# Building per-expert row lists block by block, in place of one sort at the end, in a fused attention, dense and expert kernel

## The reference

```python
# 1 local attention: 4 batches, 8 heads, 768 positions, 64 wide
for each chunk of 32 positions:
    keys = 8 memory keys + the chunk, 16 positions before it, 8 behind it
    a = softmax(q_chunk @ keys.T / 8);  out_chunk = a @ values
x = out as [3072, 512]
# 2 dense layer: w_in 512x2048, w_out 2048x512
h = x @ w_in;  x = (h * cos(h)) @ w_out
# 3 routed experts: 8 experts, w1[e] 512x1024, w2[e] 1024x512
rows = x @ w_skip > 0                   # the other rows stay as they are
e = argmax(x @ w_gate);  gate = softmax(x @ w_gate)[e]
out[rows] = x[rows] + gate * (relu(x[rows] @ w1[e]) @ w2[e])
```

## Time and profile before

| what | value |
|---|---|
| median of 3 runs | 877.75 us (876.94 to 879.12) |
| the profiled execution | 877.95 us, its span 876.3 us |
| mean granted TensorE clock | 0.973 |
| PE busy | 819.5 us, 94% of the span |
| DVE, ACT, POOL busy | 520.9, 469.0, 50.2 us |
| chain that ended last | PE 87%, DVE 5%, ACT 2%, DMA 2%, issue 2% |
| SP's loads of raw expert weights | 512 KB each, 5.6 us to landing |

### The profile page before, as it was taken

One profiled execution on the slowest core, in us unless ns is written; L12 is line 12 of the kernel. 1 busy time (PEld: TensorE's weight loads), 2 busy tenths in 40 slices (PEclk: granted clock), 3 DMA queues, 4 the chain that ended last, 5 costly groups with the idle time before them and its releaser, 6 DMA issues.

```text
span 876.3 us, 20405 instructions
## 1 busy us (share of the span) xinstructions
PE 819.5 (94%) x8018; PEld 725.3 (83%) x8019; DVE 520.9 (59%) x1030; ACT 469.0 (54%) x809; POOL 50.2 (6%) x57
## 2 busy tenths in 40 slices
PE   5799999999999999999999999999982989999995
PEld 3688888898888888888888888898961878999994
DVE  3677655655565655556555655654458577666664
ACT  3577665565566555555655565563461555444442
POOL 0000000000000000000000000000014022111110
PEclk9799999999999999999999999999995899999998
DMA  9822031104213210422132031020053375655653
GB/s 337 298 82 68 25 109 62 61 25 134 65 58 106 65 61 27 119 76 61 60 111 61 26 108 62 25 73 1 1 195 89 128 279 193 215 201 224 231 205 118
DMA packets 40690, 97.42 MB, mean 111 GB/s; under 512 B 5852, under 2 KB 5852, under 8 KB 40608
## 3 DMA queue, kind: packets, MB, share of 16 engines
q1 hardware_dynamic: 37632, 90.21, 30.3%
q0 software_dynamic: 2976, 6.05, 1.9%
HBM read 82.34 MB, written 16.79 MB: 113 GB/s over the span
## 4 chain that ended last, share of the span: by engine, by line
PE 87%; DVE 5%; ACT 2%; DMA 2%; issue 2%; POOL 0%; SPq 0%; POOLq 0%; DVEq 0%; ACTq 0%
PE h_ps L721 30%; PE y_ps L735 29%; PE h_ps L822 9%; PE y_ps L837 7%; PE s_ps L625 2%; PE s_ps L662 2%; PE turn L686 1%; PE turn L676 1%; DMA xg<-x_mid,idx_from 1%; PE turn L640 1%; DMA k_pre<-qk 1%; PE turn L696 1%; DVE w_lo L1262 1%; PE turn L807 1%; PE s_ps L807 0%
## 5 line engine op out<-in xcount | busy, mean ns | idle before, releaser
L721 PE MATMUL h_ps<-xT_hi,in_hi 128*128 128x384 f32 x512 | 181.5, 354 | 1.7 <-DVE xT_lo L1067 1.4
L721 PE MATMUL h_ps<-xT_hi,in_lo 128*128 128x384 f32 x512 | 173.5, 339 | 0.0
L721 PE MATMUL h_ps<-xT_lo,in_hi 128*128 128x384 f32 x512 | 173.0, 338 | 0.0
L735 PE MATMUL y_ps<-out_hi,g_hi 128*128 128x512 f32 x384 | 150.0, 391 | 5.0 <-DVE g_lo L1144 5.0
L735 PE MATMUL y_ps<-out_hi,g_lo 128*128 128x512 f32 x384 | 152.1, 396 | 0.0
L735 PE MATMUL y_ps<-out_lo,g_hi 128*128 128x512 f32 x384 | 151.6, 395 | 0.0
L901 ACT ACTIVATE hs<-h_ps 128x384 f32<-128x384 f32 x128 | 62.5, 488 | 156.1 <-PE h_ps L721 155.9
L1138 DVE TENSOR_SCALAR whole<-us 128x384 f32<-128x384 f32 x128 | 45.3, 354 | 131.8 <-ACT us L902 131.8
L925 ACT ACTIVATE us<-us 128x384 f32<-128x384 f32 x128 | 67.2, 525 | 73.2 <-DVE us L1140 72.9
L721 PEld LDWEIGHTS h_ps<-xT_hi,in_hi 128*128 128x128 f32 x512 | 97.2, 190 | 5.3 <-DVE xT_lo L1067 1.8
L721 PEld LDWEIGHTS h_ps<-xT_lo,in_hi 128*128 128x128 f32 x512 | 97.4, 190 | 1.6
(11 more groups left out here) (156 smaller groups left out, 1209.3 us busy)
## 6 DMA issues: line engine op xcount, KB each, us to landing
raw<-w SPq DMA_DIRECT2D x72, 512.0 KB, 5.6
k_sb<-qk SPq DMA_DIRECT2D x22, 512.0 KB, 4.5
v_sb<-v SPq DMA_DIRECT2D x22, 512.0 KB, 3.5
x_mid<-x SPq DMA_DIRECT2D x24, 256.0 KB, 5.2
out<-x SPq DMA_DIRECT2D x24, 256.0 KB, 5.6
q_sb<-qk SPq DMA_DIRECT2D x22, 256.0 KB, 3.1
in_raw<-w_in SPq DMA_DIRECT2D x4, 1024.0 KB, 14.0
out_raw<-w_out SPq DMA_DIRECT2D x4, 1024.0 KB, 15.0
```

The costliest lines, as they stand in the source:

```text
L721: last = pe.matmul(h_ps[:, f % 2, 0:BN], w[:, dc, f * P:(f + 1) * P], x[:, half, dc, :], start=(n == 0), stop=(n == 3 * DC - 1))
L735: last = pe.matmul(y_ps[:, j, :], g[:, f % RING, j * P:(j + 1) * P], w[:, f, :], start=(f == 0 and n == 0), stop=(f == FT - 1 and n == 2))
```

## The change

1. **Row lists per block.** The router's sites gain two steps. `ranks` (PE, 9 small bf16 matmuls) counts, for each row of the block just routed, the rows of the same expert ahead of it in the block; `place` (DVE, 5 steps) adds `filled_to`, the running count of each expert, and gives each row its place in a list. POOL then scatters (token, gate) pairs of 8 bytes to these places in an HBM table `lists`, 3072 places for each expert. Gates are no longer stored in `x_mid`. The router of block 6 runs early in block 7 (`ROUTER_LAST`).
2. **One-hot first slot.** The global sort is gone. Slot 0's rows of blocks 0 to 6 are gathered during block 7. Rows of block 7 are still in SBUF, and are added by 12 float32 matmuls with a one-hot matrix `hot`, in the bank in which 8 matmuls have turned the gathered ones. After block 7 POOL scatters its pairs, loads the 8 lists (`listed`), gathers slot 1, and gathers slot 0 again for the residual.
3. **Slots.** The first slot of each expert is written out; further slots of an expert are in `more_slots`, a loop that is empty here. The raw weights have two buffers. Conversion of the next slot's w1 starts within the present slot, group by group. The branch on the row count is read between the halves. `turn_rows(1)` moves behind the half of slot 0.
4. **Dense blocks** are written out, with no loop.
5. **Prologue and block 0.** `PROLOGUE` is in another order, weights are converted in pieces of 128 columns or rows, and SP's first loads are in another order.

```diff
+ROUTER = [..., (28, "route", 0), (29, "rexp", 0), (30, "gate", 0), (30, "ranks", 0), (31, "place", 0)]
+ROUTER_LAST = [..., (10, "logits", 2), (10, "route", 0), (11, "rexp", 0), (12, "gate", 0), (12, "ranks", 0), (13, "place", 0)]
-SPLIT_FIRST = 3
+AHEAD = 3
 # blocks
-            with eng.Fori(1, NB - 1) as i:
-                run(2 * i, 0)
-                run(2 * i + 1, 1)
+            for B in range(BLOCKS):
+                run(B, B % 2)
 # SP
-                wait(sp, w1lo_done, 4 * s)
+                wait(sp, w1lo_done, 4 * (s - 1))
+                    sp.dma_start(raw1[par][:, n, :], ...
 # POOL, once a block
+            def sort(R):
+                for j in range(BT):
+                    wait(pool, pairs_st[j], 16 * R)
+                pool.tensor_copy(pairs[:, :, 0:1].bitcast(I32), token[:, :].unsqueeze(2))
+                pool.tensor_scalar(token[:, :], token[:, :], float(BN), None, ALU.add)
+                pool.wait_ge(route_step, ROUTE * (R + 1))
+                for j in range(BT):
+                    pool.indirect_dma_start(out=lists[:, :], out_offset=...place[:, j:j + 1], in_=pairs[:, j, :])
 # POOL, behind block 7
+            sort(BLOCKS - 1)
+            for n in range(BT):
+                pool.wait_ge(pairs_st[n], 16 * BLOCKS)
+            for s in (1, 0):
+                load_list(s, s * N, list_ld[s])
+            for s in range(2, E):
+                load_list(s, s * N, lists_ld)
+            pool.wait_ge(list_ld[1], 16)
+            gather(1, 1, 1)
+            pool.wait_ge(list_ld[0], 32)
+            pool.wait_ge(xg_full, 2)
+            gather(0, 0, 0)
+            pool.wait_ge(lists_ld, 16 * (E - 2))
 # PE
+            def ranks():
+                for t in range(BT):
+                    for before in range(t):
+                        pe.matmul(turn[:, 0, t * E:(t + 1) * E], ones[:, :], chosen[:, before, :], ...)
+                    pe.matmul(turn[:, 0, t * E:(t + 1) * E], preceding[:, :], chosen[:, t, :], ...)
+                for t in range(BT):
+                    last = pe.matmul(turn[:, 0, BT * E:(BT + 1) * E], ones[:, :], chosen[:, t, :], ...)
+            def run_slot(s, par):
+                up_slot(s)
+                if 1 <= s < E - 1:
+                    turn_rows(s + 1, 1 - par)
+                wait(pe, o_done, 2 * s - 1)
+                half(s, 0)
+                if s == 0:
+                    turn_rows(1, 1)
+                second_half(s)
 # ACT and DVE, w1 of the next slot
+                    if following and g >= 2:
+                        w1_high(s + 1, 1 - par, g - 2)
 # DVE
+                if step == "place":
+                        then(dve.tensor_tensor(place_e, turn[:, 0, 0:BT * E], filled_to, ALU.add))
+                        then(dve.tensor_tensor(place_e, place_e, chosen, ALU.mult))
+                        then(dve.tensor_reduce(place_f, place_e, AX.X, ALU.add))
+                        then(dve.tensor_tensor(place, place_f, nowhere, ALU.add))
+                        then(dve.tensor_tensor(filled_to, filled_to, turn[:, 0, BT * E:(BT + 1) * E], ALU.add))
+            def finish(s, par, a, where):
+                dve.wait_ge(ey_full, 2 * s + a + 1)
+                if isinstance(s, int) and s == 0:
+                    dve.wait_ge(xg_ld[0], rows_landed(0, 0))
+                dve.scalar_tensor_tensor(o_sb[:, a, :], y_ps[:, a, :], listed[:, where, a, 1:2], xg[par][:, a, :], ...)
```

More of the change, by code:

```diff
@@ L572, in gather, with load_list @@
+            for R in range(BLOCKS - 1):
+                sort(R)
+            def load_list(s, first, landed):
+                pool.dma_start(listed[:, s, :, :], lists[first:first + SLOT, :].rearrange("(a p) c -> p a c", p=P)
+                               ).then_inc(landed, 16)
+            def gather(s, par, where, stored=N):
                 for a in range(2):
                     pool.indirect_dma_start(
-                        out=xg[:, par, a, :], out_offset=None, in_=x_mid[:, :],
-                        in_offset=bass.IndirectOffsetOnAxis(ap=idx_from[:, par, a:a + 1], axis=0),
@@ L593, in _ @@
+            slots(pool, run_slot)
+            used = more_slots(pool, run_more)
             for a in range(2):
@@ L799, in _ @@
-            last.then_inc(lookup_full, 1)
+            pe.wait_ge(xg_ld[0], 32)
+            pe.wait_ge(last_lg_done, BT)
+            for dc in range(DC):
+                for a in range(2):
+                    c = (dc % 2) * SLOT + a * P
+                    pe.matmul(s_ps[:, dc // 2, c:c + P], xg[0][:, a, dc * P:(dc + 1) * P], ident[:, :],
+                              start=(dc % 2 == 0 and a == 0), stop=False)
+            pe.wait_ge(route_step, ROUTE * (BLOCKS - 1) + CHOSEN)
+            ranks().then_inc(last_ranks_full, 1)
@@ L801, in turn_rows @@
+            for i in range(2):
+                for j in range(BT):
+                    if i == 0:
+                        pe.wait_ge(hot_done, j + 2)
+                    for dc in (2 * i, 2 * i + 1):
+                        c = (dc % 2) * SLOT
+                        last = pe.matmul(s_ps[:, i, c:c + SLOT], x1[:, j, dc * P:(dc + 1) * P], hot[:, j, :],
+                                         start=False, stop=(j == BT - 1 and dc % 2 == 1))
+                last.then_inc(xg_full, 1)
             def turn_rows(s, par):
-                pe.wait_ge(gathered[par], 16 * (s + 2 - par))
+                pe.wait_ge(xg_ld[par], rows_landed(s, par))
@@ L1084, in route @@
                     dve.tensor_copy(lg[:, j, :], turn[:, 0, 0:NL]).then_inc(t_free, 1)
-                elif step in ("route", "gate"):
+                elif step in ("route", "gate", "place"):
                     R = B - 1
                     n = ROUTE * R
-                    k = [0 if step == "route" else ROUTE - 3]
+                    last_one = isinstance(B, int) and B == BLOCKS
+                    k = [{"route": 0, "gate": CHOSEN + (6 if last_one else 1), "place": CHOSEN + (1 if last_one else 4)}[step]]
+                    bc = [P, BT, E]
                     def then(ins):
@@ L1124, in site @@
             def site(B, half, todo, n):
                 for step, j in todo.get(n, []):
-                    if step in ("x1", "logits", "route", "gate"):
+                    if step in ("x1", "logits", "route", "gate", "place"):
                         route(B, step, j)
```

708 lines of the change are left out of this document (411 added, 297 removed).

## The result

The changed kernel takes 874.70 us (median of 20 runs, 870.57 to 877.53), the kernel before on the same chips 878.65 us (20 runs, 876.94 to 881.05). The ratio is 0.9954, with a 95% interval from 0.9945 to 0.9963: faster, by 4 us. The forecast was 864, and 874.7 lies above the range given, 855 to 872. The direction was right, the size was over three times too large.

A forecast was written before the change was run, and what follows sets the result against it. PE's own work was taken to bound the dense blocks after block 0 and slots 2 to 7. Terms -14.5 - 0.9 + 0.5 + 4.5 - 2.0 - 1.0 = -13.4 gave 864.3 us, range 855 to 872.

The forecast's parts named there:

- the cost of `ranks` in the dense blocks: Dense blocks: PE gains seven times `ranks`, some 0.65 us each, with nothing to hide it: +4.5 us (2.1 to 7).
- my fourth rival: Dense blocks, slower: `ranks` in PE's list waits for DVE's `chosen`; one step late is 4.2 us; chance 0.02.
- -2.0: Prologue: exponentials and sums ahead of `values` remove a stall of 1.95 us: -2.0 us (-0.5 to -6.4).
- -1.0: Block 0: pieces of 128 columns halve the conversions ahead of `g_lo`: -1.0 us (0 to -3).
- Slot 1's chain: Between the stages: POOL's scatters, list loads and gathers hold slot 1's `up` until 690; slot 2 starts 14.5 us earlier.
- the landing of the pairs: Before slot 1: the scattered pairs land after 3 us, near the gate stores' median 2.7 (bounds 2.4 and 6.9).
- Rows late: Before slot 1: SP's early weight loads saturate DMA while pairs and lists travel; slot 1 at 697.5, +7.5 us; chance 0.17.
- PE's idle time: Before slot 1's `up`: PE is idle for 5.6 us after the turn, and 2.2 us is charged for the clock.
- Slots 2 to 7: Later slots stay PE's own work: one turn goes, -0.9 us; reading the row count between halves costs +0.5.
- Unrolling: Dense blocks written out: PE lost only 0.2 us in 560 with the loop, so nothing is in the sum.

The follow-up runs named there:

- the run with all six edits: Changed kernel with `ranks` one site later, slot 1's rows ahead of `o_sb`, lists behind gathers, weights held, guarded loop, gathers ahead of scatters: 859.01 us, 0.9773.

## Why the prediction was wrong

**The step whose mechanism failed** was the cost of `ranks` in the dense blocks, "+4.5 (2.1 to 7)", "with nothing to hide it". It was priced as work and came as a wait. The work is 0.32 a block, half of the 0.65 charged, and 0.80 a block is the wait for the bank. The code of `ranks` waits for two things, the free bank and `chosen`, and I worked out only the second: that `chosen` is done some 4 us ahead was right (4.6 in block 1). The release of `turn` by the transposes of site 29 was not looked at, though the trace before had it, in the block of the earlier trace rows:

```profile
573.95 0.69 DVE L1067 TENSOR_TENSOR xT_lo<-turn,xT_hi 128x512 fp32r<-128x512 f32 x1 [2.15 <-ACT xT_hi L884]
```

DVE reads that bank until 574.64, and PE comes to the site at 573.82, 0.82 earlier. The measured +6.3 of these blocks is inside the bounds given, by luck. It was my fourth rival in kind (PE stands at `ranks`), with another releaser and a fifth of its price.

**Prologue and block 0**, "-2.0" and "-1.0": +0.6 together, where executions of the same code differ by up to 1.7 in block 0. By size this is the largest miss, 3.6 us. Of the first gain 0.55 came, of the second nothing. The stall of 1.95 before `values` of the third tile stands in the changed kernel as it did before, so that the new order did not remove it. PE's waits for `g_lo` went from 4.5 to 5.3 and did not shrink with the smaller pieces. The run with the old order puts the worth of the whole part at 1 us, give or take 1.3. Why the stall stays was not tried.

**Slot 1's chain**, "-14.5" to slot 2: -13.25. The mechanism held: `up` of slot 0 at 14.51 behind the dense stage where 14.3 was forecast; the gate done at 667.1, 6.8 later than forecast with a stage that ended 6.9 later; `o_sb` behind the second gather; half clock. One term was mis-sized: the landing of the pairs, 3 taken from the median of the gate's stores, 6.7 to 7.8 measured. That is the case "Rows late" with its cause, SP's early load of the second weight buffer, shown by holding it back. Slot 1's `up` came 2.3 later than forecast and not 7.5, since POOL was quicker than its ceiling: its three scatters took 4.2 us, where 6.6 were charged, and its gathers 1.0 to 1.9 each. PE's idle time was worked out wrongly beside it: by the prediction's own numbers it is 6.5 (690 less 683.5) and not 5.6. It came as 2.28 for slot 1's rows ahead of their turn, which no step names, and 5.26 behind it. The Trainium skill (DMA: Bandwidth & Descriptors, Specifications) has it that pieces under 512 bytes are read, modified and written. No run here has the same write in larger pieces to compare, but with the DMA engines idle 8 bytes a row landed in 2.1 us, so that this was not what held the pairs.

**Slots 2 to 7**, "-0.9 + 0.5": +0.36. PE's work falls by 0.65 (140.01 to 139.36), which is most of the turn that goes, the branches cost no idle time, and a wait of 1.01 for slot 3's rows takes it back. These rows are gathered behind the scatters of slot 1, which wait for its `o_sb`: from slot 2's `up` on, the two gathers start after 4.98 and 7.17, where it was 3.72 and 5.07 before. With the gathers ahead of the scatters, in the run with all six edits, PE doesn't wait there; that edit was not tried alone.

**The end**, not in the sum: +2.11. The prediction took the stretch behind the last matmul as unchanged, because its scatter is. The empty loop that now stands behind it was not weighed. Two runs show that it is the loop.

**Unrolling** at nothing was nearly right: 0.5 us. The row of 0.2 that I used is PE's wait, and the block's length shows the rest. The Trainium skill's rule on taken branches (Runtime: NRT & Kernel Launch, Instruction fetch mechanics) agrees in direction: the one turn of the loop costs half a microsecond. Whether that is fetching, and what part of the 2.1 of the loop at the end is, no run measures apart.

The misses add up: 3.6 (prologue and block 0), 1.8 (blocks 1 to 7), 1.25 (up to slot 2), 0.8 (slots 2 to 7) and 2.1 (the end) are the 9.5 us between the forecast change of -13.4 and the measured -3.9 on the profiled clock.

## What to carry to other kernels

For an instruction that is put into the stream of the bounding engine, list every semaphore it waits for, the free buffer as well as its data, and read off the trace when each would be given; one site further the same nine matmuls cost a quarter or so (0.32 us in place of 1.1). A second buffer lets a load start early, and what it collides with then are the small transfers of the chain that decides: hold the bulk load until they have landed, and look what the held load makes late in turn. Count what stands behind the last work too: an empty loop there cost 2.1 us. When two traces differ by about 1 us, find the wait that makes the difference before you give it to the edit.

## What the runs showed of the hardware

- 8-byte rows written by an indirect DMA landed after 2.1 us with the DMA engines idle, and after 6.7 to 7.8 with them at 346 to 420 GB/s.
- An idle stretch of PE of 1.40 us left the granted clock at 1.00 (slot 1's `up` 11.74 us); behind one of 2.01 us it was 0.57 in the next window of 4 us, and the `up` took 13.25.
- A float32 matmul with 256 columns took 0.45 us at full clock (12 in 5.45), nearly four times the 0.12 of the split ones.
- A loop of six empty iterations with two tests each, at the end of the engines' lists, held the end back by 2.1 us; one branch around it cost nothing that can be seen.
